# DeltaNet and two MLPs on one core: right-hand sides and kept halves of two tiles in one operation, keys and queries loaded and multiplied apart in the opening

## The reference

```python
# attention: B, H, S, D = 4, 8, 768, 48; k_n is k over its norm
for t in range(S):
    y[:, :, t] = q_t @ state
    state = state + beta_t * outer(k_t, v_t - k_t @ state)
x = y as [3072, 384]
x = ((x @ w1) * (x @ w2)) @ w3 @ w_out          # 384 -> 1024 -> 1024 -> 384
h = x @ w_in                                    # 384 -> 1024
solu = h * softmax(h)
out = layernorm(solu) * g_ln @ w_out2           # 1024 -> 384
```

## Time and profile before

| | |
|---|---|
| Median of 3 runs | 785.2 us (782.42 to 785.26) |
| Profiled execution | 785.01 us, its span 782.9 us |
| Mean granted TensorE clock | 0.993 of 2.4 GHz |
| PE busy | 758.2 us (97% of the span) |
| DVE, ACT, POOL busy | 457.7, 347.6, 64.4 us |
| PE idle, 0 to 70 us | 7.2 us |
| PE idle, 70 to 140 us | 3.0 us |
| PE idle, 140 to 420 us | 7.1 us |

### The profile page before, as it was taken

How to read it: one execution, slowest core, us unless ns; L and a number is a source line. 1 busy time by engine, 2 the same in 40 slices (tenths; PEclk the granted TensorE clock), 3 DMA queues, 4 the chain that set the end, 5 groups by cost and what they waited for, 6 DMA issues and landing times.

```text
span 782.9 us, 22421 instructions
## 1 busy us (share of the span) xinstructions
PE 758.2 (97%) x9594; PEld 684.0 (87%) x9594; DVE 457.7 (58%) x782; ACT 347.6 (44%) x750; POOL 64.4 (8%) x96
## 2 busy tenths in 40 slices
PE   7999899999999999999999999999999999999997
PEld 6567799989989998998999888888899999999987
DVE  2955945974794598388522354443366656665663
ACT  5745346235434623634234344444344444445443
POOL 1560200100010010001000000000000000000000
PEclk9999999999999999999999999999999999999999
DMA  9940460342035025103101476540000000000001
GB/s 296 396 103 23 106 163 30 70 110 83 30 83 150 30 69 139 54 30 117 42 30 44 155 242 192 159 147 1 1 21 21 22 22 22 23 23 21 21 20 31
DMA packets 37551, 65.38 MB, mean 84 GB/s; under 512 B 3992, under 2 KB 26648, under 8 KB 36504
## 3 DMA queue, kind: packets, MB, share of 16 engines
q1 hardware_dynamic: 34760, 58.48, 25.3%
q10 hardware_dynamic: 2704, 5.60, 2.3%
HBM read 45.19 MB, written 18.87 MB: 82 GB/s over the span
## 4 chain that ended last, share of the span: by engine, by line
PE 84%; DVE 7%; DMA 3%; ACT 2%; issue 2%; SPq 0%; DVEq 0%
PE ps L1422 24%; PE ps L542 13%; PE ps L506 13%; PE ps L519 12%; PE ps L1322 5%; PE ps L1378 3%; DVE tmp L970 3%; PE ps L531 3%; PE ps L1380 3%; PE ps L1334 3%; DMA vs<-in_vtok 2%; PE ps L1435 2%; PE ps L1391 2%; PE ps L1351 1%; DVE rr L1025 1%
## 5 line engine op out<-in xcount | busy, mean ns | idle before, releaser
L1227 ACT COPY asb<-ps 128x256 f32<-128x256 f32 x96 | 35.8, 373 | 154.3 <-PE ps L1422 153.5
L1044 DVE TENSOR_TENSOR msb<-asb,ps 128x256 f32<-128x256 f32 x96 | 39.9, 415 | 87.3 <-ACT asb L1227 82.1
L542 PE MATMUL ps<-woh,uth 128*128 128x384 f32 x192 | 64.7, 337 | 0.5 <-DVE utl L459 0.5
L542 PE MATMUL ps<-woh,utl 128*128 128x384 f32 x192 | 64.5, 336 | 0.0
L542 PE MATMUL ps<-wol,uth 128*128 128x384 f32 x192 | 64.3, 335 | 0.0
L1422 PE MATMUL ps<-xh,w1h 128*128 128x256 f32 x288 | 57.3, 308 | 6.6 <-DVE msb L1044 6.6
L894 DVE TENSOR_TENSOR pt<-ps,mask 128x512 f32<-128x512 f32 x24 | 16.6, 690 | 77.2 <-ACT a L1172 77.2
L459 DVE TENSOR_TENSOR utl<-ps,uth 128x512 fp32r<-128x512 f32 x48 | 31.1, 687 | 47.9 <-ACT uth L349 47.9
L335 ACT ACTIVATE e<-ps,stats 128x1024 f32<-128x1024 f32 x24 | 26.8, 1117 | 67.6 <-DVE stats L425 67.6
L506 PE MATMUL ps<-mh,w34h 128*128 128x512 f32 x144 | 56.0, 389 | 0.0
L506 PE MATMUL ps<-ml,w34h 128*128 128x512 f32 x144 | 56.0, 389 | 0.0
(11 more groups left out here) (155 smaller groups left out, 1744.5 us busy)
## 6 DMA issues: line engine op xcount, KB each, us to landing
m_dram<-msb SPq DMA_DIRECT2D x42, 256.0 KB, 2.1
mrest<-m_dram SPq DMA_DIRECT2D x36, 256.0 KB, 5.9
kqs<-in_kq SPq DMA_DIRECT2D x20, 384.0 KB, 7.4
vs<-in_vtok SPq DMA_DIRECT2D x6, 768.0 KB, 11.0
ks<-in_ktok SPq DMA_DIRECT2D x5, 768.0 KB, 7.0
mfirst<-m_dram SPq DMA_DIRECT2D x12, 256.0 KB, 5.6
out<-wst SPq DMA_DIRECT2D x12, 192.0 KB
out<-wst SPq DMA_DIRECT2D x48, 48.0 KB, 1.5
```

What stands on the lines that cost most here:

```text
L542: ins = pe.matmul(ob[s], xx[:, j, k, :], w[:, 4 * j + k, :], start=(j == 0 and k == 0 and p == 0), stop=(j == 1 and k == 3 and p == 2))
L1044: dve.tensor_tensor(msb[:, f // 2 % 2, f % 2, :], asb[:, f % 2, :], bbank[f % 2], ALU.mult).then_inc(product, 1)
L1227: act.copy(asb[:, f % 2, :], abank[f % 2]).then_inc(a_kept, 1)
```

## The change

Three things change. First, `right_hand`, `right_hand2` and `keep_u` handle both tiles, and all 128 partitions, in one operation of 128x768 over two PSUM banks (`both`), in place of two operations of 128x384 or four of 32x384; only the first `keep_u` keeps its four. Second, keys and queries lie apart in `kqs`, so in the opening keys can be loaded and multiplied first (`first_grams`, 64 columns in place of 128) and queries later; the queries' grams come after the third block of `w3_wout`, and their masks after `stationary`. Third, the order around group 0 is changed: transfers, `FILLS`, `WARM`, the high parts of weights 8 to 15 (now in the slots 1 to 4 of group 0), `grams(1, 0)` and its copies (now behind the first `apply_inverse` and `keep_u`), and on DVE `eights_first` and `eights_products` of group 1 (now behind `right_hand`).

```diff
-        kqs = buf("kqs", [P, 2, TPG, H, P])
+        kqs = buf("kqs", [P, 2, TPG, 2, H, C])
+        both = ps[:, 0:NP, 0:DM]
-        FILLS = {(0, 0): 3, (0, 1): 3, (0, 2): 3, (0, 3): 3, (0, 4): 3, (0, 5): 3, (0, 6): 2, (0, 7): 2, (1, 0): 2}
+        FILLS = {(0, 0): 6, (0, 1): 4, (0, 2): 3, (0, 3): 3, (0, 4): 2, (0, 5): 2, (0, 6): 1, (0, 7): 1, (1, 0): 2}
-        WARM = 9
+        WARM = 6
...
+            def right_hand(n, par, tt):
+                dve.wait_ge(ks_done, TPG * n + NP * tt)
...
+                dve.tensor_tensor(rr[:, :, :], of_both(par, tt), both, ALU.subtract).then_inc(rhs, NP)
+            def right_hand2(n, tt):
+                q = TPG * n + NP * tt
+                dve.wait_ge(cross, q + NP)
+                given = of_both(0, 0) if q < NP else rr[:, :, :]
+                dve.tensor_tensor(rr[:, :, :], given, both, ALU.subtract).then_inc(rhs2, NP)
...
-                if ahead:
+                if ahead and n > 0:
                     eights_first(n + 1)
                 low_x(n, 0, 0)
                 low_x(n, 0, 1)
...
+                right_hand(n, par, 1)
+                if n == 0:
+                    eights_first(n + 1)
+                    eights_products(n + 1)
                 if ahead:
                     eights_sums(n + 1)
...
-            for tile in range(3):
-                keep_pt(0, 0, tile, first_gbank[tile])
             system_rows(0)
...
-            keep_pt(0, 0, 3, first_gbank[3])
+            for tile in range(TPG):
+                keep_first_pt(tile)
...
+            def keep_u(q, half, done, kept):
+                act.wait_ge(done, q + NP)
...
+                else:
+                    ins = act.copy(uu[:, :, :], both)
+                ins.then_inc(kept, NP)
...
-            keep_gram(0, 0, first_gbank[0])
...
+            for tile in range(TPG):
+                keep_diagonal(0, tile, first_a[tile])
+            keep_corner(0, 0, first_a[0])
+            keep_corner(0, 1, first_a[1])
             roots(0)
...
+            def first_grams(part, tile, bank, done):
+                for h in range(H):
+                    for bb in range(2):
+                        r = slice(64 * bb, 64 * bb + D)
+                        ins = pe.matmul(bank[64 * bb:64 * bb + C, h, :], kqs[r, 0, tile, 0, h, :],
+                                        kqs[r, 0, tile, part, h, :], start=True, stop=True)
+                ins.then_inc(done, 1)
...
-                        ins = pe.matmul(gbank[64 * bb:64 * bb + C, h, :], kqs[r, par, tile, h, 0:C],
-                                        kqs[r, par, tile, h, :], start=True, stop=True)
+                        ins = pe.matmul(gbank[64 * bb:64 * bb + C, h, :], kqs[r, par, tile, 0, h, :],
+                                        kqs[r, par, tile, :, h, :], start=True, stop=True)
...
-                    if early:
+                    if early and n > 0:
                         grams(n + 1, 0)
...
                     apply_inverse(n, par, tt, 0, rhs, u1_done)
+                    if early and n == 0:
+                        grams(n + 1, 0)
```

More of the change, by code:

```diff
@@ L1009, in stationary, with of_both @@
                               xt[:, :, :].rearrange("p j i -> p i j")).then_inc(inverse, 1)
[L1011 to L1026, removed]
+            def of_both(par, tt):
+                return vs[:, par, NP * tt * DM:NP * (tt + 1) * DM].rearrange("p (g n) -> p g n", n=DM)
+            def right_hand(n, par, tt):
+                dve.wait_ge(ks_done, TPG * n + NP * tt)
+                if n == 0:
+                    dve.wait_ge(v_first, 2)
+                else:
+                    dve.wait_ge(v_scaled, n)
+                dve.tensor_tensor(rr[:, :, :], of_both(par, tt), both, ALU.subtract).then_inc(rhs, NP)
[4 more added lines that the diff above has]
+                dve.tensor_tensor(rr[:, :, :], given, both, ALU.subtract).then_inc(rhs2, NP)
             def low_x(n, tt, g):
@@ L1173, in keep_corner, with keep_gram @@
                 ins.then_inc(gram_kept, 1)
[L1175 removed]
+            def keep_gram(n, tile):
                 keep_diagonal(n, tile, gbank)
                 keep_corner(n, tile, gbank)
[L1179 to L1180 removed]
+            def keep_u(q, half, done, kept):
+                act.wait_ge(done, q + NP)
                 if q == 0 and half == 0:
                     act.wait_ge(w_low, 2 * NP)
[L1183 to L1186 removed]
+                    for g in range(NP):
+                        for bb in range(2):
+                            rows = half_rows(bb, g, half)
+                            ins = act.copy(uu[rows, g, :], chain[g][rows, :])
+                else:
+                    ins = act.copy(uu[:, :, :], both)
+                ins.then_inc(kept, NP)
             def keep_y(q, g):
@@ L1245, in a_of @@
                                 keep_w34(f)
+                        if n == 0 and tt == 0 and 1 <= slot < 5:
+                            for j in range(KF + 2 * slot - 2, KF + 2 * slot):
+                                high_w(j)
                     a_of(0)
-                    if early:
+                    if early and n > 0:
                         keep_gram(n + 1, 0)
-                    keep_u(q, 0, 0, u1_done, u1_kept)
-                    keep_u(q + 1, 1, 0, u1_done, u1_kept)
+                    keep_u(q, 0, u1_done, u1_kept)
+                    if early and n == 0:
+                        keep_gram(n + 1, 0)
                     a_of(1)
@@ L1377, in outputs @@
                         if q >= NP:
-                            pe.matmul(chain[g][r, hc(h)], kqs[rk, par, tile, h, C:P], st[rk, g, hc(h)],
+                            pe.matmul(chain[g][r, hc(h)], kqs[rk, par, tile, 1, h, :], st[rk, g, hc(h)],
                                       start=True, stop=False)
@@ L1489, in tensor @@
             for tile in range(TPG):
-                grams(0, tile, first_gbank[tile])
-            pe.wait_ge(gram_kept, 1)
-            pe.wait_ge(pt_made, 1)
+                pe.wait_ge(k_first[tile // 2], 32)
+                first_grams(0, tile, first_a[tile], gram)
             for half in range(2):
@@ L1497, in tensor @@
                 w3_wout(f, range(KF))
-            pe.wait_ge(gram_kept, 3)
-            pe.wait_ge(pt_made, 3)
+                if f == 2:
+                    for tile in range(TPG):
+                        pe.wait_ge(q_first[tile // 2], 32)
+                        if tile >= 2:
+                            pe.wait_ge(gram_kept, tile + 1)
+                        first_grams(1, tile, first_p[tile], p_gram)
+            pe.wait_ge(gram_kept, TPG)
             for n in range(NG):
```

134 lines of the change are left out of this document (69 added, 65 removed).

## The result

The changed kernel takes 773.99 us (median of 4 runs, 773.46 to 775.14), the kernel before, on the same chip, 785.05 us (4 runs, 782.42 to 785.26). The ratio is 0.9869 with a 95% interval of 0.9844 to 0.9893: faster by 11.1 us, where I had forecast 779.0 in a range of 775 to 783. Profiled, it took 773.58 us with a span of 771.9, against 785.01 and 782.9.

What follows compares the result with a forecast made beforehand. PE, busy for 97% of the span, was taken as the bound, so only its idle stretches, clock and work could move the time. Gains of 5.2 and 0.7 us made 5.9 off 785.01; forecast 779.0, range 775 to 783.

Steps and rivals of the forecast that it cites:

- Part 1: Second halves of groups 1 to 4: one operation for both tiles shortens PE's waits for `multiply`; 5.2 us with the clock.
- group 2 its 0.16: Second half of group 2: the gain is the whole wait PE showed there for `multiply`, 0.16 us.
- Each `right_hand2` saves 1.32: DVE in the second halves: one operation of 0.94 us replaces four taking 2.26, saving 1.32 us.
- Part 2: Opening and group 0: keys loaded first, `w_out` lands earlier, order changed; net gain 0.7 us.
- so I keep the 1.7 us of slow clock: Opening: PE still idles 2 to 3 us before `w3_wout`, so the 1.7 us lost to slow clock stay.
- X: Opening: end of the first `apply_inverse`, where the chain starts after the change; predicted at 48.6 us, 0.8 later than Y.
- Y: Group 0 in the kernel before: start of `grams(1, 0)` at 47.83 us, from which a chain through ACT and DVE sets the time.
- (a): Rival: `w_out` lands at 13.6 us, or group 0's new 1.8 us wait brings 1.2 GHz; 782 us, chance 0.20.
- (c): Rival: grams of groups 1 to 5 read split columns more slowly; 789 us at 25% slower, chance 0.06.
- (d): Rival: an operation over two banks costs as much as the four, groups 1 to 4 keep waits; 784 us, chance 0.05.
- (b): Rival: L970 goes first in all groups, the opening's clock fall vanishes, T is 11; 775 us, chance 0.14.
- T: Opening: start of `w3_wout` once `w_out` has landed; predicted at 12 us, 11.6 at best, 13.6 at worst.

Runs made afterwards that it cites:

- rh2_only: The kernel before, with `right_hand2` alone made one operation: 777.42 us, ratio 0.9922.
- before_again: The kernel before, unchanged, measured and profiled a second time: 784.25 us, ratio 1.0007.
- merged_only: The kernel before, with the three merged operations alone (`right_hand`, `right_hand2`, `keep_u`), opening and orders left as they were: 776.35 us, ratio 0.9907.
- after: The changed kernel in its first measurement, against the kernel before: 773.99 us, ratio 0.9869; profiled 773.58 us.
- after_again: The changed kernel, unchanged, measured and profiled a second time: 773.74 us, ratio 0.9865 to the kernel before.
- opening_only: The changed kernel with `right_hand` split in two operations, `right_hand2` and `keep_u` in four, as before: 784.52 us, ratio 1.0005 to the kernel before.
- products_first: The changed kernel, with products of slots 1 and 2 ahead of group 1's `below_first` in group 0's second half: 774.1 us, ratio 0.9868.
- wo_on_sp: The changed kernel with `w_out`'s first part on SP's queue behind the first block of `w3`: 778.7 us, ratio 0.994 to the kernel before.
- scale_late: The changed kernel, with POOL's `scale_v` waiting for the large multiplication of `below_first`: 773.54 us, ratio 0.9867 to the kernel before.
- warm9: The changed kernel with nine warming matmuls in place of six: 774.07 us, ratio 0.9871 to the kernel before.
- eights_back: The changed kernel with group 1's `eights_first` and `eights_products` in their old places on DVE: 778.44 us, ratio 0.9927 to the kernel before.
- best: `products_first`, with POOL's `scale_v` also waiting for the large multiplication of `below_first`: 771.81 us, ratio 0.9845 to the kernel before.
- before: The kernel before, without the change, in its first measurement: 785.05 us; profiled 785.01 us.
- keepu_only: The kernel before, with `keep_u` alone made one copy of 128x768 (but for the first): 784.33 us, ratio 1.001.

## Why the prediction was off

I had 5.9 us of gain, and the span became 11.0 us shorter. The 5.1 us that are missing in the sum are 1.95 in Part 1, 2.0 in the opening and 1.1 behind group 4.

**The mechanism of Part 1 was right.** One operation of 128x768 takes 0.95 us (I had 0.94), ACT's change gives nothing, DVE goes first in group 1 (1.36 us in place of 3.63) and stays blocked in groups 2 to 4, and the fall of the clock at 161 us went with the wait of group 1. `rh2_only` shows that it is `right_hand2` that carries it. The sizes:

- Group 1: 1.80 predicted, 1.95 measured.
- Group 2: "group 2 its 0.16" was the step that failed. I took the wait in the row for the whole of what the group could give. PE had stalled 1.09 us just ahead, for which the profile names no releaser, and that stall lay inside the time for which it would have waited anyway; `before_again` shows 1.47 in the same place with the same length of the group. Measured: 1.24, and the 1.48 of the clock besides (68.60 against 67.12 in a group without it). The 1.24 us come only where the stall is gone, as in the changed kernel: `merged_only` and `rh2_only` still have it and took 67.23 and 67.18 us in this group, so they gained the clock's 1.4 and nothing more.
- Groups 3 and 4: 0.9 each predicted, 1.25 and 1.23 measured. "Each `right_hand2` saves 1.32" counted the operations' lengths; by starts it is 1.42, with two shorter hand-overs 1.66; the block of 0.4 that I took from it measured 0.45.
- The clock at 160: 1.4 predicted, 1.48 measured.

In sum 7.15 us where I had 5.2.

**Part 2: the step that failed is "so I keep the 1.7 us of slow clock".** X was to be 48.6 and was 46.76. `w3_wout` started at 10.71 (12 predicted, 11.6 my best case), a second wait of 1.05 that I had not seen took most of that back, and the 1.7 us of slow clock did not come: PE idled 1.59 and 1.05 us, not "2 to 3". The first part of `w_out` landed 8.8 us after its issue (13.8 before), while keys and transfers behind them moved at 398 GB/s from 6 to 10 us, where I had reckoned with 237. The rest followed the plan. `apply_inverse` came at X + 30.4 (31.0 predicted), the new waits were 1.56 and 0.92 (1.8 and 0.5 predicted), and from X to the fourth `up` 1.64 us less than from Y (47.83), where I had 1.5. Opening: 2.71 us where I had 0.7, and nearly all the difference is X (1.07 us earlier than Y, where I had 0.8 later).

Was that luck? In part. The 14 profiled executions show how waits and falls go together. The longest wait of `w3_wout` for `w_out` was 2.62 to 4.37 us in the five with the old opening, and the clock fell behind it in each. With the new opening it was 0.72 to 1.59 us in the six without a fall there (`after`, `after_again`, `opening_only`, `products_first`, `wo_on_sp`, `scale_late`), and 1.86, 2.10 and 2.14 in the three with one (`warm9`, `eights_back`, `best`). So in the opening every execution with a wait of 1.86 us or more had the fall and none with 1.59 or less, and the new opening has the short waits in six of nine. That is how the executions fell out and not a test: `wo_on_sp` was to lengthen the wait and did not, and `warm9` changed what PE did before and came out with a wait of 1.86. The eight runs of the changed kernel lie between 773.23 and 775.14 us, so luck of this kind is worth 1.9 us at most between them. For a short wait I had no row: the wait I could read was of 3.57 us.

**Behind group 4** I had expected nothing. The wait at the transition to the second MLP grew from 1.79 to 2.10 us (at 433.37; 0.3 given back), but the kernel before had a fall behind it that cost 1.46 us: from 442.92 to the end it took 340.0 us, and in `before_again`, without the fall, 338.5 from 443.28. The changed kernel needed 338.5 from 433.37. From that `up` to the end four of the 14 profiled executions took 340.0 us (`before`, `opening_only`, `products_first`, `wo_on_sp`) and ten took 338.5 to 338.6, with old and new kernels in both. So this part of the difference between the two profiles (1.1 us) belongs to their executions and not to the change. By the medians the change is worth 11.1 us, and 10.5 in the second measurement.

The rivals: (a), a worse opening, (c), slower reads of split grams (they stayed at 1.96 us a tile), and (d), merged operations as dear as before, did not happen. Of (b) the clock and the early T came true, and DVE first in all groups didn't. Its 775 came nearest, with one of its three conditions missing, since groups 2 to 4 gave more than I had read from the rows.

The Trainium skill ("SBUF — State Buffer", section "Who interferes with whom") says that the order of issue decides whether DVE or GpSimd blocks. All 14 traces agree in groups 1 to 4. Group 1 after, with DVE at 146.34 and POOL at 146.57, had 1.36 us on DVE and 3.76 on POOL; in group 2, with POOL at 211.79 and DVE at 211.92, it was 2.77 on POOL and 3.73 on DVE; `scale_late`, with POOL held back, had 1.22 us in every group.

**The stalls without a releaser** stand inside an `apply_inverse` in group 2 of four profiled executions and in group 4 of `opening_only`, and in front of the `up` behind the first `apply_inverse` of group 1 in `products_first` and `best`. The profile's list of DMA queues has one of kind `instruction`; this is its row on the page of `products_first` (packets, MB, share):

```profile
q8 instruction: 72, 1.18, 0.7%
```

That is one transfer of 16 KB every 11 us on average. Ahead of each stall the last of them stands 2.4 to 2.9 us before PE goes on:

| Execution | q8 transfer at, us | PE goes on at, us | between |
|---|---|---|---|
| `before`, group 2 | 224.35 | 227.10 | 2.75 |
| `keepu_only`, group 2 | 224.20 | 227.05 | 2.85 |
| `merged_only`, group 2 | 220.60 | 223.39 | 2.79 |
| `rh2_only`, group 2 | 221.65 | 224.42 | 2.77 |
| `opening_only`, group 4 | 359.05 | 361.46 | 2.41 |
| `products_first`, group 1 | 108.80 | 111.46 | 2.66 |
| `best`, group 1 | 108.35 | 110.90 | 2.55 |

Where it came earlier there was no stall. In `before_again` it stands at 219.50, just ahead of data transfers that fill the queues until 224.4, and PE did not stop in that `apply_inverse` (226.40); in `before` the same transfer stands at 224.35, behind such a stretch (219.0 to 223.9). In group 1 of the changed kernel it stands at 108.05, and the `up` starts at 111.26, 3.2 us later, without a wait. The nearest without a wait is `warm9` with 2.84 us (111.55 and 114.39), and `scale_late` with 2.42 (114.50 and 116.92) has a gap of 0.2 us at the same place. So the rows point to PE's own instructions coming late behind data transfers. No run tests it, for instance by moving those transfers.

**What stays open**: whether late instructions are the cause of these stalls; what the 2.1 us are by which the median of `wo_on_sp` lies above its profiled execution; and why the clock falls behind some waits of 1.8 to 2.4 us and not behind others.

## What to carry to other kernels

Size a wait by its whole group: take the time between two milestones in several groups, since a stall without a releaser can hide most of the wait that stands behind it (0.16 in the row, 1.24 us gained where the stall was gone too). Count a chain by the starts of its instructions, with the hand-overs, and not by lengths. When a change is made of parts that feed the same engine's list, price them together: here the opening alone gave nothing, the operations alone 7 us, both 11. Of the 3.2 us between the profiles of `merged_only` and the changed kernel 2.07 lie in group 0, and 1.35 in group 2, where the stall is missing.

## What was not expected of the hardware

Falls of the clock are no fixed property of a wait. Later in the program, 1.80 us in front of the fourth `up` of group 1 was followed by a fall in three executions (`before`, `before_again`, `keepu_only`) and not in `opening_only`; 2.10 and 2.11 us at the transition brought none in the changed kernel, while 1.79 and 1.99 did in `before` and `opening_only`. The falls cost 1.3 to 1.7 us each, and 2.5 in the openings of `before_again` and `merged_only`. The Trainium skill ("TensorE: Matmul & The Clock Gate", Part 1, "The HAM clock gate") says of the start of a kernel that the same kernel meets the slow clock for a different number of matmuls from run to run. Behind the idle stretch of the opening it was like that here: the first 16 matmuls of `w3_wout` in the kernel before took 7.05 us in one execution and 7.91 in the other, behind waits of 3.57 and 4.11 us.

A wait of 0.17 us in the profile was worth 0.31 when the block on DVE ahead of it was taken away (`scale_late`).

An operation of 128x768 over two PSUM banks took 0.95 us on DVE and 0.80 us on ACT, where two of 128x384 had taken 1.01 to 1.18 on DVE.
